# A mixture-of-experts pair of layers on one core: the next layer's gate taken from eight extra columns of the second product

## The chip, the cores and the metric

## The reference

All sizes are fixed: batch 2, sequence 5056, width D = 256, so N = 10112 tokens; E = 8 experts with hidden width F = 1024. All data is fp32.

```python
# 1. gated recurrence over time, per channel
f = lb + (1 - lb) * sigmoid(f_logit);  h = f * h + (1 - f) * x;  y[:, t] = h
# 2. first expert layer: router on normalised rows
logits = (x / |x|) @ (emb / |emb|).T / tau
out = gate * (relu(x @ w1[e]) @ w2[e])          # e = argmax(logits), gate = softmax at e
# 3. second expert layer: router on the first layer's output
logits = x @ w_gate                             # x is the output of layer 1, w_gate is 256 x 8
out = gate * (relu(x @ w1b[e]) @ w2b[e])
```

The output of the first expert layer for one token is a scalar gate times `h @ w2[e]`, where h is the hidden row of 1024. The second router multiplies this by `w_gate`.

## The kernel before, in words

**Stage A, the recurrence.** The tokens go by in 20 chunks of up to 512. TensorE turns the rows of x and f_logit (L1210), VectorE scans (L389), TensorE turns the result back (L1223) and forms the first router's logits with 8-column matmuls (L1229). SyncE loads four chunks ahead and stores the rows.

**The first sort (`routing`, one on each engine).** VectorE finds each token's expert, TensorE counts with ones matrices (L1256, L1259; VectorE waits for them before the scans of L440), and then ten steps of up to 8 tiles each build a table that says which token stands in which slot. In each step VectorE makes one-hot tiles (`one_hots`), ScalarE scales one (`scaled`, L1085), and TensorE multiplies (`chunk`, L1247, 79 matmuls in all). The table gives 47 pairs of 128-slot tiles per layer, each pair of one expert. GpSimd gathers the rows of a pair, and the weights of the first pair are split while the table is finished.

**The pairs (`step`).** 47 pairs belong to the first expert layer and 47 to the second. Each weight and each activation is split into a high and a low part (fp32r), and each product is the sum of three. A pair takes in four quarters j: `up` is 12 matmuls of 256 columns (L1313) and `down` is 12 (L1331), so 48 + 48 for the pair. ScalarE makes the high parts (`split_w1_hi`, `split_w2_hi`, `m_hidden`), VectorE the low parts. `down` of quarters 2 and 3 is issued in the next step. `m_y` (L1141) scales the result into `yb`, and SyncE stores it.

**The second router, before.** Only in the first layer, each of the two tiles of a pair is turned again by two transposes (`turn_y`, L1351), copied by ScalarE (`m_yT`, L1148), multiplied with `w_gate` by two fp32 matmuls of 8 columns (`y_logits`, L1342; each stands as two records in the trace), and the 8 logits are copied by VectorE (`m_logits`, L690).

**The second sort (`resort`).** It runs in small portions, one at each `tick`, beside the pairs: part 0 for the first 32 pairs' tokens, part 1 for the rest. `FRONT` is the number of portions before the table steps.

Every engine's order of work is the order in which the code is written. The order between engines is kept by semaphores. Bank numbers: 0 and 1 take `up`, 4 the turned input, 5 the second router, 6 and 7 `down`.

## Time and profile before

| what | value |
|---|---|
| median of 3 runs | 1382.06 us (1380.33 to 1382.55) |
| the profiled execution: its time | 1380.53 us |
| its span, first to last instruction | 1378.8 us |
| TensorE busy | 1326.5 us, 96% |
| VectorE, ScalarE, GpSimd busy | 971.3, 836.0, 440.5 us |
| mean granted TensorE clock | 0.974 |

Busy time of TensorE holds overlaps and modelled ends, so the starts of rows are the safer measure of its pace. A row of the timeline gives the start, the time from the first start to the last end, the engine, the line, the operation with its tiles, and how many instructions the row merges. "Idle before" stands in brackets with what ended it. The stages are: stage A to 110 us, the first sort to 166 us, the pairs of the first layer, then the pairs of the second, and the last scatter at the end.

### The profile page before, as it was taken

How to read it: one execution, taken by the hardware profiler on the slowest of the kernel's cores; microseconds unless marked ns; L12 is line 12 of the kernel's file. 1: busy time of each engine (PE TensorE's matmuls, PEld its weight loads, DVE VectorE, ACT ScalarE, POOL GpSimd, SP SyncE). 2: the span in 40 equal slices, each digit the busy share in tenths (PEclk: the TensorE clock that was granted, in tenths of full speed). 3: DMA queues.
4: the chain of work that ended last, by engine and by line, in shares of the span. 5: the costliest groups of instructions: out<-in, count | busy, mean ns of one | idle time of the engine just before them, and what ended most of it. 6: DMA issues, size and time to landing. Idle time of an engine off the chain costs nothing.

```text
span 1378.8 us, 31340 instructions
## 1 busy us (share of the span) xinstructions
PE 1326.5 (96%) x11005; PEld 1296.1 (94%) x11005; DVE 971.3 (70%) x1468; ACT 836.0 (61%) x1402; POOL 440.5 (32%) x458
## 2 busy tenths in 40 slices
PE   7994799999999999999999999999999999999996
PEld 6892499999999999999999999899999999999996
DVE  5888476666666666679876679777777777777773
ACT  5774266666666666666656665556666666666663
POOL 4572222121121221222112144324444444444431
PEclk9995599999999999999999999999999999999998
DMA  7984686656665665668856657446666666666650
GB/s 275 327 273 93 90 260 198 202 199 193 217 198 191 210 199 195 199 204 142 262 157 201 212 194 229 162 154 221 221 217 213 222 224 217 224 214 217 223 185 1
DMA packets 189559, 276.83 MB, mean 201 GB/s; under 512 B 33351, under 2 KB 151765, under 8 KB 189493
## 3 DMA queue, kind: packets, MB, share of 16 engines
q1 hardware_dynamic: 175956, 240.74, 56.5%
q0 software_dynamic: 13536, 35.21, 7.7%
q8 instruction: 41, 0.67, 0.2%
q14 instruction: 26, 0.20, 0.0%
HBM read 242.69 MB, written 35.18 MB: 202 GB/s over the span
## 4 chain that ended last, share of the span: by engine, by line
PE 89%; DVE 6%; issue 2%; POOL 1%; ACT 1%; DMA 1%; SPq 0%; DVEq 0%; POOLq 0%; ACTq 0%
PE bank L1313 38%; PE bank L1331 37%; PE bank L1247 4%; PE bank L1297 3%; PE bank L1342 2%; PE bank L1351 1%; PE bank L1229 1%; PE bank L1210 1%; PE bank L1223 1%; DVE hT L389 1%; DVE gx L379 1%; DVE w1l L363 1%; POOL fg L894 1%; DVE hl L675 0%; DMA fin<-in_f_logit 0%
## 5 line engine op out<-in xcount | busy, mean ns | idle before, releaser
L1313 PE MATMUL bank<-xs,w1h 128*128 128x256 f32 x3008 | 570.3, 288 | 1.5 <-DVE xs L664 1.5
L1125 ACT ACTIVATE hh<-bank 128x512 fp32r<-128x512 f32 x376 | 225.3, 599 | 413.2 <-PE bank L1313 385.1
L1313 PEld LDWEIGHTS bank<-xs,w1h 128*128 128x128 f32 x3008 | 461.3, 189 | 3.2 <-DVE xs L664 1.9
L675 DVE SCALAR_TENSOR_TENSOR hl<-bank,hh 128x512 fp32r<-128x512 f32 x376 | 259.9, 691 | 249.3 <-ACT hh L1125 246.3
L1331 PE MATMUL bank<-w2h,hl 128*128 128x256 f32 x1504 | 423.1, 281 | 0.0
L1331 PE MATMUL bank<-w2l,hh 128*128 128x256 f32 x1504 | 422.4, 281 | 0.0
L1331 PE MATMUL bank<-w2h,hh 128*128 128x256 f32 x1504 | 421.7, 280 | 0.0
L1313 PE MATMUL bank<-xs,w1l 128*128 128x256 f32 x1504 | 421.5, 280 | 0.0
L1313 PEld LDWEIGHTS bank<-xs,w1l 128*128 128x128 f32 x1504 | 283.6, 189 | 0.0
L1331 PEld LDWEIGHTS bank<-w2h,hh 128*128 128x128 f32 x1504 | 283.3, 188 | 0.0
L1331 PEld LDWEIGHTS bank<-w2l,hh 128*128 128x128 f32 x1504 | 283.0, 188 | 0.0
L1331 PEld LDWEIGHTS bank<-w2h,hl 128*128 128x128 f32 x1504 | 283.0, 188 | 0.0
L363 DVE TENSOR_TENSOR w1l<-w1raw,w1h 128x1024 fp32r<-128x1024 f32 x188 | 230.2, 1225 | 44.7 <-ACT w1h L1038 44.6
L370 DVE TENSOR_TENSOR w2l<-w2raw,w2h 128x1024 fp32r<-128x1024 f32 x188 | 230.2, 1225 | 43.2 <-ACT w2h L1046 28.1
L972 POOL DMA_INDIRECT xb<-rows_a,row_i x94 | 110.1, 1172 | 459.2 <-DVE meta L668 440.9
L982 POOL DMA_INDIRECT out_y<-yb,tok x94 | 125.8, 1338 | 312.2 <-DVE tok L683 282.0
L1038 ACT ACTIVATE w1h<-w1raw 128x1024 fp32r<-128x1024 f32 x188 | 197.5, 1051 | 7.3 <-DMA w1raw<-in_moe_w 7.3
L1046 ACT ACTIVATE w2h<-w2raw 128x1024 fp32r<-128x1024 f32 x188 | 197.6, 1052 | 0.8 <-DMA w2raw<-in_moe_w 0.8
L972 POOL DMA_INDIRECT xb<-rows_b,row_i x94 | 108.9, 1159 | 67.0 <-DVE meta L668 29.7
L1141 ACT ACTIVATE yb<-bank,meta 128x256 f32<-128x256 f32 x188 | 78.7, 471 | 11.4 <-PE bank L1331 4.5
L664 DVE TENSOR_TENSOR xs<-bank,xs 128x512 fp32r<-128x512 f32 x94 | 64.9, 690 | 11.7 <-ACT xs L1119 9.5
L1247 PE MATMUL bank<-vals,lane_oh 128*128 128x124 bf16 (+2 forms) x237 | 59.3, 414 | 10.8 <-DVE vals L519 10.8
(160 smaller groups left out, 1033.8 us busy)
## 6 DMA issues: line engine op xcount, KB each, us to landing
w1raw<-in_moe_w SPq DMA_DIRECT2D x94, 1024.0 KB
w2raw<-in_moe_w SPq DMA_DIRECT2D x94, 1024.0 KB, 5.5
rows_b<-yb SPq DMA_DIRECT2D x94, 128.0 KB, 2.1
xin<-in_x SPq DMA_DIRECT2D x19, 512.0 KB, 5.5
fin<-in_f_logit SPq DMA_DIRECT2D x19, 512.0 KB, 7.2
rows_a<-h_rows SPq DMA_DIRECT2D x19, 512.0 KB, 5.2
xb<-rows_a,row_i POOLq DMA_INDIRECT x94, 4.3
xb<-rows_b,row_i POOLq DMA_INDIRECT x94, 5.5
```

Source lines behind the costliest of these rows:

```text
L363: v.tensor_tensor(w1l[:, par(i), cols], w1raw[:, par(i), cols], w1h[:, par(i), cols].bitcast(fp32), ALU.subtract).then_inc(w1_lo, 1)
L370: v.tensor_tensor(w2l[:, par(i), cols], w2raw[:, par(i), cols], w2h[:, par(i), cols].bitcast(fp32), ALU.subtract).then_inc(w2_lo, 1)
L675: v.scalar_tensor_tensor(hl[:, j, :], bank[j % UB][:, :], 0.0, hh[:, j, :].bitcast(fp32), ALU.max, ALU.subtract).then_inc(hid_lo, 1)
L972: pool.indirect_dma_start(xb[:, s, :], None, rows_of(i), bass.IndirectOffsetOnAxis(row_i[:, s:s + 1], 0)).then_inc(x_in[s], 16)
L982: pool.indirect_dma_start(out, bass.IndirectOffsetOnAxis(tok[:, s:s + 1], 0), yb[:, s, :], None, bounds_check=N - 1, oob_is_err=False).the ...
L1038: nc.scalar.activation(w1h[:, par(i), cols], w1raw[:, par(i), cols], ACT.Copy).then_inc(w1_hi, 1)
L1046: nc.scalar.activation(w2h[:, par(i), cols], w2raw[:, par(i), cols], ACT.Copy).then_inc(w2_hi, 1)
L1125: nc.scalar.activation(hh[:, j, :], bank[j % UB][:, :], ACT.Relu).then_inc(hid_hi, 1)
L1141: nc.scalar.activation(yb[:, s, :], bank[Y_BANK + par(i)][:, t * D:(t + 1) * D], ACT.Copy, scale=meta[:, bass.ds(in_layer(i).value(2 * G, ...
L1247: ins = mm(bank[b][:, 0:2 * W], lane_oh[:, g % RS, :, t], vals[:, g % RS, 0:2 * W, t], start=first and t == 0, stop=last and t == w - 1)
L1313: ins = mm(bank[j % UB][:, f * GW:(f + 1) * GW], w[:, p, o:o + P], xs[:, p, a, c * GW:(c + 1) * GW], start=k == 0, stop=k == 3 * DC - 1)
L1331: ins = mm(bank[Y_BANK + p][:, t * D:(t + 1) * D], a[:, j, f * GW + t * P:f * GW + (t + 1) * P], w[:, p, o:o + D], start=(j, t, f, k) == ( ...
```

## The change

The product of each expert's `w2` (1024 x 256) with `w_gate` (256 x 8) is formed once, in the first sort. The result, 1024 x 8 per expert, goes to DRAM (`gates_d`) and is loaded for each pair of the first layer beside `w2`, is split into a high and a low part, and stands as columns 256 to 263 of `w2h` and `w2l`. The 48 `down` matmuls of a first-layer pair have 264 columns instead of 256, and the extra 8 columns are the second router's logits before the gate factor. `turn_y`, `m_yT` and `y_logits` are gone, and `m_logits` copies both tiles' logits from `yb` at once.

The work of the first sort is cut into 16 units, two per expert. A unit is `turn_w2`, 8 transposes of 128 columns, two ScalarE copies of 512 columns (`keep_turned`), and `gate_w2`, 8 fp32 matmuls of 8 columns. Four units are begun ahead of the counting matmuls (`EARLY`), six between these and the table (`SPREAD`), one after each third table step, and the rest behind the table. Seven of the eight `w2` matrices are loaded from the last chunks of stage A on, in addition to the weights of the first pair, and the eighth after the store of the pair table. The first pair's weights are split by ScalarE behind the table steps, where before they were split ahead of them.

Since `down` now takes four banks (4 to 7), `resort` counts and builds its table in one bank (2), by 4 experts at a time in part 0 and by 2 in part 1; both parts begin one step earlier, and `FRONT` of part 1 goes from 15 to 19.

```diff
+    DX = D + E
+    EW = FC * E
+    WUNITS = 2 * E
+    EARLY, SPREAD = 4, 6
...
+        w2_stage = [sb(f"w2_stage{n}", [P, WE], fp32, gate_only) for n in range(5)]
+        w2_turn = sb("w2_turn", [P, 2 * DC * 512], fp32, gate_only)
...
-        X_BANK, L_BANK, Y_BANK = 4, 5, 6
-        CUM_BANK, SUM_BANK = 2, 3
+        S_BANK, X_BANK, Y_BANK = 2, 3, 4
+        w2_all = [w1raw[:, 1, :], w2raw[:, 1, :]] + w2_stage + w2_stage[0:1]
+        T_BANK, TAB_BANK = [5, 7], 4
+        W_BANK = [6, S_BANK]
...
-                if i.var is None and i.const * JS + j >= XA * JS + 2 * JS:
-                    next(part0 if i.const < NP + 2 else part1, None)
+                if i.var is None and i.const >= XA + 1:
+                    next(part0 if i.const < NP + 1 else part1, None)
...
-        FRONT = [18, 15]
+        FRONT = [18, 19]
+        EXPERTS_AT_ONCE = [4, 2]
...
+                if i.var is None and NCH - 5 <= i.const < NCH - 1:
+                    load_all(i.const - (NCH - 5))
                 if i.var is None and i.const == NCH - 1:
+                    load_all(4)
                     load_w1(Index(0))
                     load_w2(Index(0))
+                    load_all(5)
+                    load_all(6)
...
+            load_all(E - 1)
+            store_gates(0)
+            sp.wait_ge(gate_out, 16)
+            load_wg(Index(0))
             sp.wait_ge(dve_c, mark["experts"])
             read_expert(Index(1))
+            sp.wait_ge(w2_turned, 4 * DC)
             load_w1(Index(1))
             load_w2(Index(1))
+            load_wg(Index(1))
...
+            def keep_turned(u):
+
+                wait(act, gate_ok, u - 1)
+                for c in range(DC):
+                    act.wait_ge(w2_turned, 2 * u + c + 1)
+                    o = (2 * (u % 2) + c) * 512
+                    nc.scalar.activation(w2_turn[:, o:o + 512], bank[T_BANK[c]][:, :],
+                                         ACT.Copy).then_inc(w2t_ok, 1)

...
+                for u in range(EARLY):
+                    keep_turned(u)
                 act.wait_ge(lg_ok, NCH)
                 act.wait_ge(shift_ok, 2)
                 nc.scalar.activation(ex[:, 0:TT, :], shifted[:, 0:TT, :], ACT.Exp).then_inc(act_s, 1)
+                for u in range(EARLY, EARLY + SPREAD):
+                    keep_turned(u)
+                    if u == EH * 2:
+                        keep_gates(0)
+                u = EARLY + SPREAD
                 for q, t0 in enumerate(range(0, TT, RC)):
                     scaled(q, min(RC, TT - t0), ST)
+                    if q % 3 == 2:
+                        keep_turned(u)
+                        u += 1
+                for c in range(DC):
+                    split_w1_hi(Index(0), c)
+                for u in range(u, WUNITS):
+                    keep_turned(u)
+                for half in range(2):
+                    split_w2_hi(Index(0), half)
+                keep_gates(1)
...
+                    n = DX if layer_of(i) == 0 else D
+                    nc.scalar.activation(yb[:, s, 0:n], bank[Y_BANK + s][:, 0:n], ACT.Copy,
                                          scale=meta[:, bass.ds(in_layer(i).value(2 * G, 2 * t), 1)]
                                          ).then_inc(y_ok, 1)
-
-            def m_yT(i, t):
-
-                wait(act, y_turned, i.value(G, t + 1))
-                nc.scalar.activation(yT[:, t, :], bank[L_BANK][:, 0:D], ACT.Copy).then_inc(yT_ok, 1)
...
+            def turn_w2(u):
+
+                e, h = divmod(u, 2)
+                if u == 0:
+                    pe.wait_ge(rows_ok, NCH)
+                if h == 0:
+                    pe.wait_ge(all_in[e], 16)
+                for c in range(DC):
+                    wait(pe, w2t_ok, 2 * (u - 1) + c + 1)
+                    for n in range(FC // 2):
+                        o = (h * (FC // 2) + n) * D + c * P
+                        ins = nc.tensor.transpose(bank[T_BANK[c]][:, n * P:(n + 1) * P],
+                                                  w2_all[e][:, o:o + P], ident[:, :])
+                    ins.then_inc(w2_turned, 1)
+
+            def gate_w2(u):
+
+                e, h = divmod(u, 2)
+                pe.wait_ge(w2t_ok, 2 * u + 2)
+                if u == 0:
+                    pe.wait_ge(lg_kept, NCH)
+                if u == EH * 2:
+                    pe.wait_ge(dve_c, mark["totals"])
+                for n in range(FC // 2):
+                    for c in range(DC):
+                        o = (2 * (u % 2) + c) * 512 + n * P
+                        col = (e % EH) * EW + (h * (FC // 2) + n) * E
+                        ins = mm(bank[W_BANK[e // EH]][:, col:col + E], w2_turn[:, o:o + P], wg_T[:, c, :],
+                                 start=c == 0, stop=c == DC - 1)
+                ins.then_inc(gate_ok, 1)
+
+            def gate_step(u):
+                if u < WUNITS:
+                    turn_w2(u)
+                if u > 0:
+                    gate_w2(u - 1)
...
             def routing():
                 T = TT
+                for u in range(EARLY):
+                    gate_step(u)
                 pe.wait_ge(dve_c, mark["oh"])
                 for b in range(2):
 
...
                     ins = mm(bank[2 + b][:, 0:EH * T], ones_b[:, :], oh[:, b * EH:(b + 1) * EH, 0:T],
                              start=True, stop=True)
                 ins.then_inc(pe_s, 1)
+                for u in range(EARLY, EARLY + SPREAD):
+                    gate_step(u)
+                u = EARLY + SPREAD
                 for q, t0 in enumerate(range(0, T, RC)):
-                    chunk(q, min(RC, T - t0), ST, 4, q == 0, t0 + RC >= T)
+                    chunk(q, min(RC, T - t0), ST, bank[TAB_BANK][:, 0:2 * ST], q == 0, t0 + RC >= T)
+                    if q % 3 == 2:
+                        gate_step(u)
+                        u += 1
+                for u in range(u, WUNITS + 1):
+                    gate_step(u)
...
+                n = DX if layer_of(i) == 0 else D
                 for t in range(G):
                     for f in range(2):
                         k = 0
                         for a, w in ((hh, w2h), (hh, w2l), (hl, w2h)):
-                            o = (2 * j + f) * D
-                            ins = mm(bank[Y_BANK + p][:, t * D:(t + 1) * D],
-                                     a[:, j, f * GW + t * P:f * GW + (t + 1) * P], w[:, p, o:o + D],
-                                     start=(j, t, f, k) == (0, 0, 0, 0), stop=(j, f, k) == (JS - 1, 1, 2),
-                                     skip_group_check=True)
+                            ins = mm(bank[Y_BANK + rows_slot(i, t)][:, 0:n],
+                                     a[:, j, f * GW + t * P:f * GW + (t + 1) * P], w[p][:, 2 * j + f, 0:n],
+                                     start=(j, f, k) == (0, 0, 0), stop=(j, f, k) == (JS - 1, 1, 2))
                             k += 1
...
-            def y_logits(i, t):
-
-                wait(pe, yT_ok, i.value(G, t + 1))
-                for c in range(DC):
-                    ins = mm(bank[L_BANK][:, D:D + E], yT[:, t, c * P:(c + 1) * P],
-                             wg_T[:, c, :], start=c == 0, stop=c == DC - 1)
-                ins.then_inc(ylg_ok, 1)
-
-            def turn_y(i, t):
-                s = rows_slot(i, t)
-                wait(pe, y_ok, i.value(G, t + 1))
-                wait(pe, ylg_kept, i.value(G, t))
-                for c in range(DC):
-                    ins = nc.tensor.transpose(bank[L_BANK][:, c * P:(c + 1) * P],
-                                              yb[:, s, c * P:(c + 1) * P], ident[:, :])
-                ins.then_inc(y_turned, 1)
```

How TensorE's instructions move. First the place between stage A and the first pair, before. Rows are in the order of issue; the number at the end is how many follow each other.

```order
L1223 MATMUL bank<-ident,hT 128x128 x6
L1229 MATMUL bank<-en_T,hT 128x8 x6
L1256 MATMUL bank<-oh,upto 128x316 x2
L1259 MATMUL bank<-oh,ones_b 128x316 x2
L1247 MATMUL bank<-vals,lane_oh 128x188 x79
L1297 MATMUL bank<-ident,xb 128x128 x4
L1313 MATMUL bank<-xs,w1h 128x256 x2
L1313 MATMUL bank<-xs,w1l 128x256
```

The same place after the change, its beginning: L1340 and L1346 are the former L1223 and L1229, L1412 and L1415 the counting matmuls (L1256, L1259), L1369 is `turn_w2` and L1385 is `gate_w2`.

```order
L1340 MATMUL bank<-ident,hT 128x128 x6
L1346 MATMUL bank<-en_T,hT 128x8 x6
L1369 MATMUL bank<-ident,w1raw 128x128 x16
L1385 MATMUL bank<-wg_T,w_turn 128x8 x8
L1369 MATMUL bank<-ident,w2raw 128x128 x8
L1385 MATMUL bank<-wg_T,w_turn 128x8 x8
L1369 MATMUL bank<-ident,w2raw 128x128 x8
L1385 MATMUL bank<-wg_T,w_turn 128x8 x8
L1412 MATMUL bank<-oh,upto 128x316 x2
L1415 MATMUL bank<-oh,ones_b 128x316 x2
L1369 MATMUL bank<-ident,w_stage 128x128 x8
L1385 MATMUL bank<-wg_T,w_turn 128x8 x8
```

Two units' transposes now stand together at the start, and three units of `gate_w2` stand ahead of the counting matmuls, for which VectorE waits. Then the table steps after the change (L1401 is the former L1247):

```order
L1401 MATMUL bank<-vals,lane_oh 128x188 x24
L1369 MATMUL bank<-ident,w_stage 128x128 x8
L1385 MATMUL bank<-wg_T,w_turn 128x8 x8
L1401 MATMUL bank<-vals,lane_oh 128x188 x24
L1369 MATMUL bank<-ident,w_stage 128x128 x8
L1385 MATMUL bank<-wg_T,w_turn 128x8 x8
L1401 MATMUL bank<-vals,lane_oh 128x188 x24
L1369 MATMUL bank<-ident,w_stage 128x128 x8
L1385 MATMUL bank<-wg_T,w_turn 128x8 x8
L1401 MATMUL bank<-vals,lane_oh 128x188 x7
L1369 MATMUL bank<-ident,w_stage 128x128 x8
L1385 MATMUL bank<-wg_T,w_turn 128x8 x8
```

The 79 table matmuls are cut into 24, 24, 24 and 7. Behind the last 7 stand three `turn_w2` and four `gate_w2` in all, of which the last two rows here are the first, and then the first pair's input is turned.

The second place is a first-layer pair, where a quarter's `down` ends and the next `up` begins. Before:

```order
L1331 MATMUL bank<-w2h,hh 128x256
L1331 MATMUL bank<-w2l,hh 128x256
L1331 MATMUL bank<-w2h,hl 128x256
L1342 MATMUL bank<-wg_T,yT 128x8 x2
L1313 MATMUL bank<-xs,w1h 128x256 x2
L1313 MATMUL bank<-xs,w1l 128x256
```

After, at the corresponding place (L1496 is the former L1331, L1476 the former L1313):

```order
L1496 MATMUL bank<-w2h,hh 128x264
L1496 MATMUL bank<-w2l,hh 128x264
L1496 MATMUL bank<-w2h,hl 128x264
L1476 MATMUL bank<-xs,w1h 128x256 x2
L1476 MATMUL bank<-xs,w1l 128x256
```

The 8-column matmuls between `down` and `up` are gone, as are the transposes of L1351 at the other quarters, and the `down` matmuls are wider.

## Rows read from the trace of the kernel before

**Rows 1.** Page, parts 1 and 4: engines' busy time; the chain that ended last.

```profile
PE 1326.5 (96%) x11005; PEld 1296.1 (94%) x11005; DVE 971.3 (70%) x1468; ACT 836.0 (61%) x1402; POOL 440.5 (32%) x458
PEclk9995599999999999999999999999999999999998
PE 89%; DVE 6%; issue 2%; POOL 1%; ACT 1%; DMA 1%; SPq 0%; DVEq 0%; POOLq 0%; ACTq 0%
```

**Rows 2.** Timeline of TensorE, input transposes in layer 1, then layer 2.

```profile
260.78 0.60 PE L1297 MATMUL bank<-ident,xb 128*128 128x128 f32 x4
273.88 0.60 PE L1297 MATMUL bank<-ident,xb 128*128 128x128 f32 x4
...
1099.81 0.60 PE L1297 MATMUL bank<-ident,xb 128*128 128x128 f32 x4
1111.59 0.60 PE L1297 MATMUL bank<-ident,xb 128*128 128x128 f32 x4
```

**Rows 3.** Groups of TensorE by line: records of the second router.

```profile
L1342 PE MATMUL bank<-wg_T,yT 128*128 128x8 f32 x376 | 47.7, 235 | 0.0
L1351 PE MATMUL bank<-ident,yb 128*128 128x128 f32 x188 | 35.7, 271 | 0.0
```

**Rows 4.** Timeline of TensorE, 172 to 175 us: first and last of 12 `down` matmuls.

```profile
172.72 0.28 PE L1331 MATMUL bank<-w2h,hh 128*128 128x256 f32 x1
...
174.02 0.28 PE L1331 MATMUL bank<-w2h,hl 128*128 128x256 f32 x1
```

**Rows 5.** Timeline of TensorE, the first sort.

```profile
106.09 1.52 PE L1223 MATMUL bank<-ident,hT 128*128 128x128 f32 x6 [1.04 <-ACT sq L1069]
107.40 2.57 PE L1229 MATMUL bank<-en_T,hT 128*128 128x8 f32 x12
116.75 0.70 PE L1256 MATMUL bank<-oh,upto 128*128 128x316 bf16 x2 [6.79 <-DVE oh L427]
...
128.53 26.92 PE L1247 MATMUL bank<-vals,lane_oh 128*128 128x188 bf16 x79 [10.54 <-DVE vals L519]
...
164.10 0.69 PE L1297 MATMUL bank<-ident,xb 128*128 128x128 f32 x2 [0.84 <-DMA xb<-rows_a,row_i]
166.28 0.80 PE L1313 MATMUL bank<-xs,w1h 128*128 128x256 f32 x2 [1.48 <-DVE xs L664]
```

**Rows 6.** Windows: busy time and count by engine, granted clock, DMA.

```profile
104.00:106.00 2.00, 1.05 (x10) 0.96 (x9) 1.87 (x4) 1.94 (x9) 0.30 (x1) 0.79 0.01 4
106.00:108.00 2.00, 1.91 (x10) 1.94 (x10) 0.00 (x0) 0.36 (x1) 0.00 (x0) 0.50 0.56 190
...
148.00:150.00 2.00, 2.00 (x8) 0.87 (x6) 0.00 (x0) 0.00 (x0) 0.00 (x0) 0.50 0.00 0
...
170.00:172.00 2.00, 2.00 (x19) 2.00 (x18) 1.74 (x3) 1.72 (x3) 0.18 (x1) 1.00 1.11 369
```

**Rows 7.** Timeline of TensorE, the start of stage A.

```profile
8.33 1.08 PE L1210 MATMUL bank<-ident,xin 128*128 128x128 f32 x4 [1.02 <-DMA fin<-in_f_logit]
9.21 1.06 PE L1210 MATMUL bank<-ident,fin 128*128 128x128 f32 x4
...
16.73 1.04 PE L1223 MATMUL bank<-ident,hT 128*128 128x128 f32 x8
17.60 1.85 PE L1229 MATMUL bank<-en_T,hT 128*128 128x8 f32 x16
19.30 0.63 PE L1210 MATMUL bank<-ident,xin 128*128 128x128 f32 x4
```

**Rows 8.** Timelines of VectorE and ScalarE in and behind the first sort.

```profile
118.09 0.81 DVE L440 TENSOR_TENSOR_SCAN before<-ones_f,bank 128x316 f32<-128x316 f32 x1
...
164.83 0.60 ACT L1119 ACTIVATE xs<-bank 128x512 fp32r<-128x512 f32 x1 [18.35 <-PE bank L1297]
```

**Rows 9.** Page, part 6: DMA issues, count, size of each, us to landing.

```profile
w2raw<-in_moe_w SPq DMA_DIRECT2D x94, 1024.0 KB, 5.5
```

**Rows 10.** Timeline of TensorE, a table step of the second sort.

```profile
901.31 1.95 PE L1247 MATMUL bank<-vals,lane_oh 128*128 128x124 bf16 x8
902.91 0.59 PE L1313 MATMUL bank<-xs,w1h 128*128 128x256 f32 x2
```

More of the change, by code:

```diff
@@ L228, in build @@
         w2_in = [sem(f"w2_in{n}") for n in range(2)]
+        all_in = [sem(f"all_in{n}") for n in range(E)]
+        w2_turned = sem("w2_turned")
+        w2t_ok = sem("w2t_ok")
+        gate_ok = sem("gate_ok")
+        gate_kept = sem("gate_kept")
+        gate_out = sem("gate_out")
+        wg_in = [sem(f"wg_in{n}") for n in range(2)]
+        wg_hi = sem("wg_hi")
+        wg_lo = sem("wg_lo")
         w1_hi = sem("w1_hi")
@@ L695, in _ @@
             m_x(Index(0))
+            split_wg_lo(Index(0))
             def step(i):
-                last, last2, nxt = i.plus(-1), i.plus(-2), i.plus(1)
-                if here(last2) and layer_of(last2) == 0:
-                    m_logits(last2, 0)
+                last, nxt = i.plus(-1), i.plus(1)
                 if here(i):
@@ L725, in step @@
                         split_w2_lo(nxt, 1)
+                    if here(nxt) and layer_of(nxt) == 0:
+                        split_wg_lo(nxt)
+                if here(last) and layer_of(last) == 0:
+                    m_logits(last)
                 tick(i, 3)
@@ L1088, in routing @@
             def routing():
-                for c in range(DC):
-                    split_w1_hi(Index(0), c)
-                for half in range(2):
-                    split_w2_hi(Index(0), half)
+                for u in range(EARLY):
+                    keep_turned(u)
                 act.wait_ge(lg_ok, NCH)
@@ L1175, in step @@
                         split_w2_hi(nxt, 0)
-                if here(last) and layer_of(last) == 0:
-                    m_yT(last, 0)
                 tick(i, 2)
@@ L1239, in _, with chunk @@
             a_back(Index(NCH - 1), tiles_in(NCH - 1))
-            def chunk(g, w, W, b, first, last):
+            def turn_w2(u):
[30 more added lines that the diff above has]
+                    gate_w2(u - 1)
+            def chunk(g, w, W, table, first, last):
                 pe.wait_ge(lane_ok, g + 1)
@@ L1325, in down @@
                     wait(pe, y_ok, i.value(G, -G))
+                    if layer_of(i) == 0:
+                        wait(pe, wg_lo, i.value(1, 1))
+                n = DX if layer_of(i) == 0 else D
                 for t in range(G):
@@ L1360, in step @@
             def step(i):
[L1361 removed]
+                last, nxt = i.plus(-1), i.plus(1)
                 if here(i):
@@ L1380, in step @@
                     down(i, 0)
-                if here(last) and layer_of(last) == 0:
-                    turn_y(last, 0)
                 tick(i, 2)
@@ L1386, in step @@
                     down(i, 1)
-                if here(last) and layer_of(last) == 0:
-                    y_logits(last, 0)
                 tick(i, 3)
```

181 lines of the change are left out of this document (112 added, 69 removed).

## The prediction

> **What bounds the kernel now.** I read the page's busy times first, then the chain that ended last, then TensorE's timeline stage by stage, with the granted clock of short windows beside it. The reader is to see that TensorE is busy for 96% of the span and carries 89% of the chain that ended last, with VectorE far behind at 6% [rows 1]. So time is mostly what TensorE is given to do, and the other engines count only where TensorE waits. That is so in one place alone, the first sort. Between the end of the last 8-column matmuls of stage A, at about 109.9 us, and the first `up` matmul at 166.28, TensorE runs 79 table matmuls for 26.92 us and a few small ones, and stands idle for 6.79, then 10.54 us, and again ahead of the first pair [rows 5]. It also runs at the lower of its two clocks there: the granted clock is 0.79 over the window from 104 us, so it falls inside it, is 0.50 at 106 and still at 148, with TensorE busy through the whole window, and is back at 1.00 at 170, some 4 us into dense `up` matmuls [rows 6, 5].
>
> **What goes from the first-layer pairs.** In steady state the input transposes of two following pairs are 273.88 - 260.78 = 13.10 us apart in layer 1 and 1111.59 - 1099.81 = 11.78 us in layer 2 [rows 2]. The two layers run the same 96 wide matmuls, and the difference, 1.32 us, is the second router: four transposes (188 records over 47 pairs) and four 8-column matmuls (376 records, two each) [rows 3], with the wait for the array at each change of kind. TensorE is the limit in both, so all of it is on the path: 47 x 1.32 = 62.0 us go. ScalarE loses two copies a pair and gains one of 64 columns, VectorE exchanges two tiny copies for one and a subtraction of 64 columns. Both engines keep pace with TensorE in layer 2 at 11.78 us a pair and have about the same work as there, so I cost their edits at nothing; if that cover were gone, a late `m_y` would hold the next `down`, and would show as idle time in front of L1496. The gate load is 32 KB a pair beside 2 MB of weights, hidden likewise.
>
> **What comes to the pairs.** 47 x 48 = 2256 `down` matmuls get 8 more columns. Twelve matmuls start between 172.72 and 174.02, that is 11 gaps, 118.2 ns each for 256 columns [rows 4]. At 2.4 GHz 8 columns are 3.3 ns, and by proportion to the gap 3.7 ns. From below the bound is nothing: 256 columns at 2.4 GHz are 106.7 ns, so 11.5 ns of each gap belong to something other than columns and could hold 3.3 more. From above, no row has an fp32r matmul over 256 columns; were the last 8 columns to cost a pass of their own, the nearest row is a record of 8 columns at 0.106 us, 17.60 to 19.30 for 16 of them [rows 7], and 2256 of them 240 us. I take 3.3 ns, 7.5 us in all: it is the columns' own time, and it lies by the proportional value, which rests on the gaps of this very instruction.
>
> The Trainium skill, "TensorE: Matmul & The Clock Gate", section "Back-to-back issue gap", gives columns/2.4 + 2.5 ns, an estimate of 109.2 ns for 256 and 112.5 for 264; the trace's 118.2 does not agree in size, and the difference of 3.3 ns would give the same 7.5 us. By the page's statement on the moving operand, up to 512 columns for all types, the second pass would not come.
>
> **What comes to the first sort.** A unit is 8 transposes and 16 records of 8-column matmuls. At the lower clock six transposes take 107.40 - 106.09 = 1.31 us, 0.218 each, and 12 records take 2.57 us with the last one's own end in it, 0.20 to 0.214 each [rows 5]. A unit is then 8 x 0.218 + 16 x 0.20 = 4.94 us, and 16 units are 79.1 us. At the higher clock it is (17.60 - 16.73) for the transposes and (19.30 - 17.60) for the records, 2.57 us, or 41.1 in all [rows 7]. The four counting matmuls take 1.3 us from 116.75 to VectorE's scan at 118.09 and the table 26.9 us, at the lower clock [rows 5, 8]. TensorE works strictly in the written order, and everything stands ahead of the first pair, so the sum is a chain: 109.9 + 79.1 + 1.3 + 26.9 = 217.2 us. Behind it come the first pair's four transposes at 0.218, the ScalarE copy and the VectorE subtraction, as before: from 164.10, the last two transposes, to 166.28 it was 2.2 us, and two more transposes make 2.6. The first `up` starts at 219.8 instead of 166.28, 53.5 us later.
>
> What lies beside this chain. The counting result comes 9 to 10 us later to VectorE, whose scan began at 118.09 [rows 8]; its chain to the first table step needs 128.53 - 118.09 = 10.4 us, so the first table step is ready near 139, while TensorE is in its units until about 158. The long idle times of before are thus filled and VectorE, ScalarE and GpSimd are covered; the gather of the first rows, which cost TensorE 0.84 us of waiting [rows 5], is covered too. The eight loads of `w2` are 8 MB; one load lands 5.5 us after issue in the median [rows 9], and those for unit 2e have 10 us between them. On SyncE's queue the eighth load waits for the twelfth turned half, and the first gate load for the store of the gates; behind them stand the loads of pair 1, which wait for `experts`. VectorE writes that after the low part of the first pair's `w2`, which now waits for ScalarE behind `keep_turned(15)`: I get 216 us for the issue, 3.5 us ahead of the first `up`, where the trace of before has 3 us. So nothing is late there by more than a fraction of a microsecond. I add 1 us for the 50 or so new waits of TensorE.
>
> **The sum.** -62.0 + 7.5 + 53.5 + 1.0 = 0.0 us. The profiled execution's time of 1380.53 us, of which the span is 1378.8, stays 1380.5. The median of the runs shown, 1382.06, is 1.5 us above it. The sum would give 1382.1 there; I name 1381.0, between the two, because of the clock's short returns (below), of which one of 3 us is as likely as not. What such a kernel's measurement can tell from no change is 0.2%, 2.8 us. So the gain in the pairs is given back in a sort that ran at half clock, and the outcome hangs on three small numbers.
>
> **Rival 1: the clock comes back in the sort.** For it: in stage A the transposes of 8.33 and 9.21 are 0.22 us apart, the lower clock, and those of 16.73 0.11 us, with nothing but transposes (and two tiny ones) run in between [rows 7], so transposes alone brought the clock up; and the first two units' 16 transposes now stand in a row. In stage A a mixture of transposes and 8-column records also kept it. Against it: the table matmuls did not bring it back in 27 us without a gap [rows 5, 6]; a unit has 8 transposes to 16 records, a full chunk of stage A by its code 24 to 16, and the last chunks, where the clock fell, no more input transposes. At full clock throughout, the units are 38.0 us shorter, the counting 0.6, and the table hardly: a 124-column table matmul at full clock takes 1.60/8 = 0.20 us [rows 10], by columns 0.30 for 188 against 0.341, so 3 us. That is 1382.1 - 41.6 = 1340.5 us. Each microsecond spent at the higher clock is one gained, so it decides from 3 us on. I give 0.15 to more than 5 us.
>
> The Trainium skill, same page, "Part 4: PE-mode transpose", says that transposes do not engage the higher clock, which speaks against this rival and for the lower clock throughout. Rows 7 show the opposite for fp32 transposes in this kernel. By the page the first `up` stands at 219.8 us for certain, by the row up to 41.6 us of it can come back.
>
> **Rival 2: the 8 columns are free**, held by the 11.5 ns of each gap. Then it is 7.5 us less, 1374.6 us, still faster by more than 2.8. For it speaks only that gap; against it, that at the lower clock a table matmul of 188 columns takes 0.341 us and at the higher one of 124 columns 0.20 [rows 5, 10], so width is paid for in both. 0.12.
>
> **Rival 3, slower: TensorE waits for ScalarE's copies.** `gate_w2` of a unit needs both copies, and the next but one `turn_w2` the bank. A copy of 512 columns takes 0.60 us [rows 8]. Between the transposes of a unit and its matmuls stand the next unit's transposes, 1.7 us, which cover it; but ScalarE also has the ten scalings of the table and one copy of the gates in the same order, and the records' upper value of 0.214 works in the same direction. A wait of one copy a unit is 16 x 0.60 = 9.6 us, 1391.7 us. It decides from 0.19 us a unit on, a unit of over 5.1 us. 0.16. The second pass of the 8 columns, +240 us, gets 0.02.
>
> **How the numbers follow.** The forecast case has 0.55; its own range is 1376 to 1386, of it 0.13 faster, 0.34 within 0.2%, 0.08 slower. With rival 1 (0.15) and 2 (0.12) faster by over 0.2% is 0.40, within is 0.34, and with rival 3 and the second pass slower is 0.26. The range 1367 to 1391 leaves out most of rival 1 and a little above, under 0.2. It takes in both ends of the records' time (+3.6 us) and of the 8 columns (-7.5 to +0.9 us).
>
> **What would show it.** The first `up` matmul (L1476) at 217 to 221 us, with L1369 at 0.22 and L1385 at 0.20 us a record and the granted clock at 0.50 from about 105 to 223; the first counting matmul (L1412) near 126 to 127; no idle time of TensorE over 1 us between 110 and 217; pairs of layer 1 at 11.78 + 48 x 0.0033 = 11.94 us, those of layer 2 unchanged; gaps of L1496 at 121.5 ns. It is wrong if the windows between 110 and 217 read 1.00 for more than a few microseconds, if the pairs of layer 1 stand at 11.78 or above 12.1 us, or if TensorE shows idle time ahead of L1385, L1401 or L1496.

## The result and the profile after

| | before | after |
|---|---|---|
| median | 1381.74 us (10 runs, 1380.21 to 1382.56) | 1385.62 us (10 runs, 1383.23 to 1387.63) |
| profiled execution, its span | 1380.53, 1378.8 us | 1385.2, 1383.5 us |
| ratio after to before | | 1.0028, 95% interval 1.0018 to 1.0038 |
| mean granted clock | 0.974 | 0.954 |

The change made the kernel slower by 3.9 us. The time lies in the predicted range, but I had named 1381 us, no change, as the likeliest, and the move is beyond the measurement's uncertainty.

The page after, parts 1 and 4. TensorE is busy 30 us longer and carries still more of the last chain [rows 1].

```profile
PE 1356.2 (98%) x10829; PEld 1326.6 (96%) x10829; DVE 974.8 (70%) x1470; ACT 825.5 (60%) x1389; POOL 428.0 (31%) x458
...
PE 91%; DVE 3%; DMA 2%; issue 1%; ACT 1%; POOL 1%; SPq 0%; ACTq 0%; DVEq 0%; POOLq 0%
```

TensorE's timeline of the first sort after, which answers to [rows 5]; columns are start, time, engine, line, operation, count.

```profile
109.56 3.75 PE L1369 MATMUL bank<-ident,w1raw 128*128 128x128 f32 x16
113.11 3.42 PE L1385 MATMUL bank<-wg_T,w_turn 128*128 128x8 f32 x16
116.39 1.95 PE L1369 MATMUL bank<-ident,w2raw 128*128 128x128 f32 x8
...
126.41 0.69 PE L1412 MATMUL bank<-oh,upto 128*128 128x316 bf16 x2
...
152.45 1.95 PE L1369 MATMUL bank<-ident,w_stage 128*128 128x128 f32 x8
154.19 3.42 PE L1385 MATMUL bank<-wg_T,w_turn 128*128 128x8 f32 x16
157.47 8.25 PE L1401 MATMUL bank<-vals,lane_oh 128*128 128x188 bf16 x24
...
217.34 1.09 PE L1460 MATMUL bank<-ident,xb 128*128 128x128 f32 x4
219.91 0.80 PE L1476 MATMUL bank<-xs,w1h 128*128 128x256 f32 x2 [1.48 <-DVE xs L713]
```

There is no idle time left ahead of the table. A unit takes 5.02 us (116.39 to 121.40 in the same timeline), and the first `up` starts at 219.91 us, 53.6 later than before. The windows after show the lower clock in the sort, which answers to [rows 6].

```profile
116.00:120.00 4.00, 4.00 (x21) 4.00 (x21) 1.75 (x3) 1.19 (x2) 2.35 (x2) 0.50 1.05 389
200.00:204.00 4.00, 4.00 (x21) 4.00 (x21) 2.10 (x2) 1.19 (x2) 3.51 (x4) 0.50 0.00 0
```

The input transposes of following pairs after, first two in layer 1 and then two in layer 2 [rows 2].

```profile
404.40 0.60 PE L1460 MATMUL bank<-ident,xb 128*128 128x128 f32 x4
416.35 0.60 PE L1460 MATMUL bank<-ident,xb 128*128 128x128 f32 x4
...
1103.78 0.60 PE L1460 MATMUL bank<-ident,xb 128*128 128x128 f32 x4
1115.60 0.60 PE L1460 MATMUL bank<-ident,xb 128*128 128x128 f32 x4
```

A pair of layer 1 takes 11.95 to 11.98 us (mean 11.967) in place of 13.09, and a pair of layer 2 takes 11.82 in place of 11.785. The first and the last of the 12 wide `down` matmuls of one quarter, which answer to [rows 4]:

```profile
433.07 0.28 PE L1496 MATMUL bank<-w2h,hh 128*128 128x264 f32 x1
...
434.41 0.28 PE L1496 MATMUL bank<-w2h,hl 128*128 128x264 f32 x1
```

That is 1.34 us for 11 gaps. The mean of 87 such quarters between 300 and 560 us is 1.337 us, 121.6 ns a gap, against 1.300 us and 118.2 ns before. To place the rest I read the same transposes at pairs 34, 43, 48, 58 and 93. Before:

```profile
601.20 0.60 PE L1297 MATMUL bank<-ident,xb 128*128 128x128 f32 x4
...
726.92 0.60 PE L1297 MATMUL bank<-ident,xb 128*128 128x128 f32 x4
...
792.38 0.60 PE L1297 MATMUL bank<-ident,xb 128*128 128x128 f32 x4
...
934.84 0.60 PE L1297 MATMUL bank<-ident,xb 128*128 128x128 f32 x4
...
1347.32 0.60 PE L1297 MATMUL bank<-ident,xb 128*128 128x128 f32 x4
```

After:

```profile
619.80 0.60 PE L1460 MATMUL bank<-ident,xb 128*128 128x128 f32 x4
...
737.88 0.60 PE L1460 MATMUL bank<-ident,xb 128*128 128x128 f32 x4
...
797.73 0.60 PE L1460 MATMUL bank<-ident,xb 128*128 128x128 f32 x4
...
938.33 0.60 PE L1460 MATMUL bank<-ident,xb 128*128 128x128 f32 x4
...
1351.97 0.60 PE L1460 MATMUL bank<-ident,xb 128*128 128x128 f32 x4
```

| stretch | before | after | difference |
|---|---|---|---|
| to the first `up` | 166.28 | 219.91 | +53.6 |
| to pair 34 | 434.9 | 399.9 | -35.0 |
| pairs 34 to 43 (part 0 of the second sort) | 125.7 | 118.1 | -7.6 |
| 43 to 48 | 65.5 | 59.9 | -5.6 |
| 48 to 58 | 142.5 | 140.6 | -1.9 |
| 58 to 93 | 412.5 | 413.6 | +1.2 |
| sum | | | +4.7 |

### The profile page after: what moved, and what is told of

The parts are those of the page before. It is cut to its first block, busy times and chain, and to the rows that moved or that the text cites. A ratio compares the mean times of both kernels' runs of the same rounds, so it can differ in the third digit from the quotient of the medians.

```text
span 1383.5 us, 31017 instructions
## 1 busy us (share of the span) xinstructions
PE 1356.2 (98%) x10829; PEld 1326.6 (96%) x10829; DVE 974.8 (70%) x1470; ACT 825.5 (60%) x1389; POOL 428.0 (31%) x458
## 4 chain that ended last, share of the span: by engine, by line
PE 91%; DVE 3%; DMA 2%; issue 1%; ACT 1%; POOL 1%; SPq 0%; ACTq 0%; DVEq 0%; POOLq 0%
PE bank L1476 38%; PE bank L1496 38%; PE bank L1401 4%; PE bank L1385 4%; PE bank L1460 3%; PE bank L1369 2%; DMA w1raw<-in_moe_w 1%; PE bank L1346 1%; PE bank L1327 1%; PE bank L1340 1%; DVE hT L434 1%; DVE gx L424 1%; POOL fg L979 1%; ACT sq L1179 0%; DMA fin<-in_f_logit 0%
## 5 line engine op out<-in xcount | busy, mean ns | idle before, releaser
L1476 PE MATMUL bank<-xs,w1h 128*128 128x256 f32 x3008 | 564.0, 286 | 1.5 <-DVE xs L713 1.5
L1476 PEld LDWEIGHTS bank<-xs,w1h 128*128 128x128 f32 x3008 | 464.8, 189 | 3.0 <-DVE xs L713 1.9
L1496 PE MATMUL bank<-w2h,hh 128*128 128x264 f32 (+1 forms) x1504 | 426.0, 283 | 0.0
L1496 PE MATMUL bank<-w2l,hh 128*128 128x264 f32 (+1 forms) x1504 | 424.8, 282 | 0.0
L1496 PE MATMUL bank<-w2h,hl 128*128 128x264 f32 (+1 forms) x1504 | 424.6, 282 | 0.0
L1476 PE MATMUL bank<-xs,w1l 128*128 128x256 f32 x1504 | 424.3, 282 | 0.0
L1476 PEld LDWEIGHTS bank<-xs,w1l 128*128 128x128 f32 x1504 | 284.5, 189 | 0.0
L1496 PEld LDWEIGHTS bank<-w2l,hh 128*128 128x128 f32 x1504 | 283.7, 189 | 0.0
L1496 PEld LDWEIGHTS bank<-w2h,hh 128*128 128x128 f32 x1504 | 283.0, 188 | 0.0
L1496 PEld LDWEIGHTS bank<-w2h,hl 128*128 128x128 f32 x1504 | 282.6, 188 | 0.0
L1057 POOL DMA_INDIRECT xb<-rows_a,row_i x94 | 99.5, 1058 | 435.5 <-DVE meta L717 417.4
L1262 ACT ACTIVATE yb<-bank,meta 128x264 f32<-128x264 f32 (+1 forms) x188 | 79.3, 474 | 12.7 <-issue 5.8
L1401 PE MATMUL bank<-vals,lane_oh 128*128 128x124 bf16 (+2 forms) x237 | 60.0, 415 | 0.7 <-DVE vals L562 0.7
```

What stands on the lines that cost most here:

```text
L1057: pool.indirect_dma_start(xb[:, s, :], None, rows_of(i), bass.IndirectOffsetOnAxis(row_i[:, s:s + 1], 0)).then_inc(x_in[s], 16)
L1262: nc.scalar.activation(yb[:, s, 0:n], bank[Y_BANK + s][:, 0:n], ACT.Copy, scale=meta[:, bass.ds(in_layer(i).value(2 * G, 2 * t), 1)]).then ...
L1401: ins = mm(table, lane_oh[:, g % RS, :, t], vals[:, g % RS, 0:2 * W, t], start=first and t == 0, stop=last and t == w - 1)
L1476: ins = mm(bank[j % UB][:, f * GW:(f + 1) * GW], w[p][:, o:o + P], xs[:, p, a, c * GW:(c + 1) * GW], start=k == 0, stop=k == 3 * DC - 1)
L1496: ins = mm(bank[Y_BANK + rows_slot(i, t)][:, 0:n], a[:, j, f * GW + t * P:f * GW + (t + 1) * P], w[p][:, 2 * j + f, 0:n], start=(j, f, k) ...
```

## The experiments

Twelve kernels ran. Times are medians, beside runs of the kernel before on the same chip.

**1. The units left out.** `turn_w2`, `keep_turned`, `gate_w2` and the loads for them are removed.

```diff
-                for u in range(EARLY):
-                    gate_step(u)
...
-                for u in range(EARLY, EARLY + SPREAD):
-                    gate_step(u)
...
-                for u in range(u, WUNITS + 1):
-                    gate_step(u)
```

> The changed kernel with all 16 units of the gate product left out of the first sort (turn_w2, keep_turned, gate_w2, and the eight w2 loads for them); the 8 extra columns are filled from 64 columns of w2 per expert, so the router's numbers are not the reference's. Theory A, the units are a chain of TensorE work of 16 x 5.02 us of which idle time of before takes some 24 us: the first input transpose comes at 162 to 164 us as before instead of 217.3, and the whole is 54 us shorter than the changed kernel, 1331.5 us. Theory B, the sort's shift is partly something else (the loads, the later split of the first weights): the first transpose comes after 168 us and the whole is over 1336 us.

Measured: 1334.9 us, ratio to before 0.9655 (0.9639 to 0.9671). The timeline of TensorE has the first input transposes at 165.20 us and the first `up` at 168.88, 2.6 us later than before and 51 to 52 us earlier than in the change:

```profile
165.20 0.66 PE L1430 MATMUL bank<-ident,xb 128*128 128x128 f32 x2 [7.19 <-DVE expert L572]
...
168.88 0.80 PE L1446 MATMUL bank<-xs,w1h 128*128 128x256 f32 x2 [1.48 <-DVE xs L713]
```

Stage A ended 2.5 us later in this execution (a short fall of the clock within it), so the sort itself is as long as before. Without the units the change would be worth 3.4%; the units cost 50.7 us by medians. Theory A holds for the sort. The total is 3.4 us over its forecast by medians and 5.0 in the profiled execution, where 2.5 us are stage A and 2.5 us the stretch from pair 34 to 43 (120.5 us, against 118.1 in the change); number 12 comes back to that stretch.

**2 and 3. More columns in `gate_w2`.** The moving operand, 8 columns of `w_gate`, is repeated 4 or 8 times. The surplus columns are overwritten or unused, the results are the same.

```diff
-                        ins = mm(bank[W_BANK[e // EH]][:, col:col + E], w2_turn[:, o:o + P], wg_T[:, c, :],
+                        ins = mm(bank[W_BANK[e // EH]][:, col:col + 8 * E].rearrange("p (r e) -> p r e", e=E),
+                                 w2_turn[:, o:o + P], wg_T[:, c, :].unsqueeze(1).to_broadcast([P, 8, E]),
                                  start=c == 0, stop=c == DC - 1)
```

> The changed kernel with the moving operand of gate_w2 repeated 4 times, 32 columns instead of 8; the results used are the same. 
Measured with 64 columns: 1366.0 us (1365.57 to 1366.91), ratio 0.9889 (0.9872 to 0.9905). TensorE's timeline of the sort:

```profile
113.93 3.52 PE L1385 MATMUL bank<-wg_T,w_turn 128*128 128x64 f32 x16
117.24 1.91 PE L1369 MATMUL bank<-ident,w2raw 128*128 128x128 f32 x8
118.94 2.23 PE L1385 MATMUL bank<-wg_T,w_turn 128*128 128x64 f32 x16
121.02 1.04 PE L1369 MATMUL bank<-ident,w2raw 128*128 128x128 f32 x8
121.89 1.90 PE L1385 MATMUL bank<-wg_T,w_turn 128*128 128x64 f32 x16
...
194.70 1.11 PE L1461 MATMUL bank<-ident,xb 128*128 128x128 f32 x4 [0.79 <-DVE empty L545]
```

The windows of the same run, clock in the third column from the end:

```profile
120.00:124.00 4.00, 4.00 (x38) 3.92 (x38) 0.00 (x0) 1.70 (x3) 0.01 (x1) 1.00 1.07 359
...
150.00:154.00 4.00, 4.00 (x19) 3.46 (x19) 0.00 (x0) 2.97 (x4) 0.00 (x0) 0.50 1.13 8
```

Eight times the columns cost nothing: 16 records take 113.93 to 117.24, 3.31 us, at the lower clock, against 3.27 with 8 columns, and 1.73 us in the higher one. The clock came up within the second unit, stayed through the following ones, a unit then taking 2.6 us, and fell at the table steps. So the time of a record does not depend on its columns between 8 and 64, and the number of columns decides whether the clock is held; that it is the weights that pace the record is not shown. The gain of 19.6 us over the change is half of theory A's upper bound because the clock is lost at the table steps and comes and goes in the last units. With 32 columns the median of eleven runs is 1375.27 us, and they fall in two groups, seven from 1366.7 to 1377.0 and four from 1387.2 to 1390.3; the ratio of the seven is 0.9939 (0.9922 to 0.9956). The profiled one is of the upper group, and its clock reads 0.50 in the sort:

```profile
120.00:124.00 4.00, 4.00 (x20) 4.00 (x21) 0.00 (x0) 0.56 (x1) 0.66 (x1) 0.50 1.07 363
```

No trace of the lower group was taken. The mean granted clock of each run is on record: 0.962 to 0.969 in the seven and 0.950 to 0.953 in the four, so the seven had the higher clock for longer, most likely in the sort.

**4. One wide product of three.**

```diff
+                            n = DX if layer_of(i) == 0 and k == 0 else D
                             ins = mm(bank[Y_BANK + rows_slot(i, t)][:, 0:n],
```

> The changed kernel with only one of the three down products (high part by high part) 264 columns wide in layer 1, the other two 256: the logits lack the low parts. Theory A, each of 2256 matmuls pays 3.7 ns for its 8 columns: 1504 of them become narrow and the kernel gains 5.6 us, 1380 us, pairs of layer 1 at 11.85 us instead of 11.97. Theory B, the price is not in the columns but in the tiles' layout or the extra bank changes: pairs of layer 1 stay at 11.95 or above, gain under 1.5 us.

Measured: 1383.35 us, ratio 1.0009 (0.9999 to 1.0020). The median is only 2.3 us under the change's, with runs spread from 1379.1 to 1385.1; in the profiled one the stretch from pair 34 to 43 takes 121.9 us, 3.8 more than in the change, which hides most of the gain. The timeline is sharper:

```profile
401.74 0.60 PE L1460 MATMUL bank<-ident,xb 128*128 128x128 f32 x4
...
425.45 0.60 PE L1460 MATMUL bank<-ident,xb 128*128 128x128 f32 x4
```

Two pairs take 23.71 us, 11.86 each, and the mean over some 25 pairs is 11.84. Against 11.967 that is 0.13 us for 32 narrower matmuls, 4.0 ns each. Theory A holds: the columns are paid for, and rival 2 is refuted. The 4.0 ns are not the price of every wide matmul, though. Over the pairs of layer 2 in the same trace, 11.82 us, the 16 that stayed wide cost about 0.02 us, hardly over 1 ns each. All 48 together cost 0.15 us a pair in the change (11.967 against 11.82), 3.1 ns each, and the gaps say 3.4.

**5 and 6. Thirteen units ahead of the table**, with 64 columns and with 8. The units between the table steps go ahead of them.

```diff
-    EARLY, SPREAD = 4, 6
+    EARLY, SPREAD = 4, 9
...
-                    if q % 3 == 2:
-                        gate_step(u)
-                        u += 1
```

> The kernel with 64 columns in gate_w2, with SPREAD = 9 and no units between table steps: 13 units ahead of the table, 3 behind it. Theory A, the granted clock is held by units of 64 columns and lost to table steps: the clock stays at 1.00 from about 120 us to the table, the three moved units take 2.6 us instead of 5.0 each, 7 us less, the first input transpose at 188 instead of 194.7, 1359 us. Theory B, the clock in the units is a matter of chance and of the window in which they fall: the gain of the 64 columns does not grow, 1366 us or more, and the runs spread by over 5 us.

> The changed kernel (8 columns in gate_w2) with the order of the fast variant: 13 units ahead of the table, 3 behind. Theory A, order alone does not bring the clock up, what streams in gate_w2 does: the sum of TensorE's work in the sort stays, first input transpose at 216 to 219 us, 1385 us. Theory B, it is the table steps between units that keep the clock down: the first transpose comes 5 us earlier or more, under 1380 us.

Measured with 64 columns: 1358.75 us, ratio 0.9832 (0.9814 to 0.9849), first transpose at 188.74 us. With 8 columns: 1386.59 us, ratio 1.0028 (1.0016 to 1.0040), no better than the change. Windows of the first (64 columns):

```profile
140.00:144.00 4.00, 4.00 (x40) 4.00 (x38) 1.15 (x3) 1.91 (x4) 0.00 (x0) 1.00 0.81 9
160.00:164.00 4.00, 4.00 (x13) 1.71 (x12) 2.06 (x4) 1.26 (x2) 0.00 (x0) 0.50 0.07 18
```

Windows of the second (8 columns), in the same place:

```profile
150.00:154.00 4.00, 4.00 (x21) 4.00 (x20) 0.00 (x0) 1.19 (x3) 0.00 (x0) 0.50 1.89 5
```

So the order alone gains nothing, and with the clock up it is worth 7 us, as theory A said in both. Number 6 has its first transposes at 218.95 us.

**7. Layer 2's 0.035 us a pair: the weights' layout.** The kernel before with separate tiles and rows of 264 elements.

```diff
-        w2h = sb("w2h", [P, 2, WE], f32r)
...
+            w2h.insert(0, sb(f"w2h{n}", [P, FC, DX], f32r))
```

> The kernel before with only the storage of the split weights as in the change: separate tiles per parity, rows of w2h and w2l 264 elements apart, hh and hl between them; all matmuls 256 columns, everything else as before. Theory A, the 0.035 us by which the pairs of layer 2 became longer (11.785 to 11.82) comes from the layout: the period here is 11.82. Theory B, it comes from the two banks of down per pair: the period here stays at 11.785.

Measured in one run: 11.783 us a pair in layer 2, 13.08 in layer 1. It is not the layout.

**8. The banks of `down`.**

```diff
...
+                                ins = mm(bank[Y_BANK + 2 * p][:, t * D:(t + 1) * D],
...
```

> The changed kernel with both tiles of a layer-2 pair in one bank again, as before the change; layer 1 unchanged. Theory A (layout): layer 2 stays at 11.82 us a pair. Theory B (banks): layer 2 is back at 11.785, layer 1 still 11.97, 1.6 us less in all.

Measured in one run: 11.818 us in layer 2, as in the change. It is not the banks; both expected causes of these two experiments are excluded.

The trace of number 8 shows something else. Its first sort is that of the change, with 8 columns in `gate_w2`, and yet the clock came up in it for some 3.6 us:

```profile
130.47 1.85 PE L1387 MATMUL bank<-wg_T,w_turn 128*128 128x8 f32 x16
132.17 1.07 PE L1371 MATMUL bank<-ident,w_stage 128*128 128x128 f32 x8
```

```profile
130.00:134.00 4.00, 4.00 (x37) 4.00 (x35) 3.59 (x14) 2.25 (x4) 0.00 (x0) 0.93 0.14 46
```

It fell again within the next unit of the same kind. In the four other traces with 8 columns, those of the change and of numbers 4, 6 and 11, it reads 0.50 through the whole sort.

**9 and 10. The address of `xs` and the bank of the turned input.** Number 9 changes both in the kernel of number 7, number 10 the banks alone.

```diff
+        apart = sb("apart", [P, 288], fp32)
...
-        X_BANK, L_BANK, Y_BANK = 4, 5, 6
-        CUM_BANK, SUM_BANK = 2, 3
+        X_BANK, L_BANK, Y_BANK = 3, 5, 6
+        CUM_BANK, SUM_BANK = 2, 4
```

> The kernel before with the weights' layout of the change, the activations xs moved to the address that they have in the change (1152 bytes further), and the turned input in bank 3 as in the change. Theory A, the addresses or the bank of the turned input make TensorE's pairs 0.035 us longer: layer 2 at 11.82 us a pair, layer 1 at 13.11. Theory B, neither: layer 2 stays at 11.785.

> The kernel before with the weights' layout of the change and the turned input in bank 3 instead of 4, with xs at its old address. Theory A, the address of xs and what lies behind it makes the pairs longer: layer 2 is at 11.785 us here. Theory B, the bank does: 11.81.

Number 9, the timeline's transposes in layer 2:

```profile
1101.81 0.60 PE L1304 MATMUL bank<-ident,xb 128*128 128x128 f32 x4
1113.62 0.60 PE L1304 MATMUL bank<-ident,xb 128*128 128x128 f32 x4
```

Number 10:

```profile
1098.80 0.60 PE L1303 MATMUL bank<-ident,xb 128*128 128x128 f32 x4
1110.58 0.60 PE L1303 MATMUL bank<-ident,xb 128*128 128x128 f32 x4
```

By means over 31 pairs, 11.813 and 11.783 us. The whole of number 9 is 3.7 us longer than that of number 10 (1383.18 and 1379.44, one run each). What lies behind the padding, from the constants to `xs` and `yb`, moved by 1152 bytes (and `yT` went elsewhere), and that makes a pair 0.03 us longer. Which tile it is was not tested, but the traces say in which matmuls the time lies: the 12 `up` matmuls of a quarter, which read `xs`, take 1.441 us in number 9 and 1.433 in number 10, the 12 `down` matmuls 1.424 in both (from first start to the start of what follows, means of over 120 quarters in layer 2). From the kernel before to the change `up` went from 1.438 to 1.444 in the same way, and `down` in layer 2 stayed at 1.42.

**11. Part 0 of the second sort one step later.**

```diff
-                if i.var is None and i.const >= XA + 1:
+                if i.var is None and i.const >= XA + 2:
```

> The changed kernel with part 0 of the second sort begun one step later, as before the change. Theory A, the 2.5 us that this part cost more than before come from TensorE's waits for VectorE (0.8 us for the one-hot tile, 0.7 for the first vals), which follow from the shorter step, not from the earlier begin: the steps 34 to 42 again cost 10.4 us over the plain pair, no change in all. Theory B, the earlier begin collides with something in that step: the excess is back at 7.9 us, 2.5 us less.

Measured in one run: 1387.97 us; pairs 34 to 43 take 118.36 us, as in the change (118.08). The begin is not the cause. That the waits follow from the shorter step is not tested by this.

**12. TensorE's part of the second sort one quarter later**, in the kernel of number 5.

```diff
                 lo, hi, T, W, p0, pairs = part_of(r)
-                for _ in range(5):
+                for _ in range(6):
                     yield
                 for b, e, k, number in groups(r):
```

> The kernel with 64 columns and 13 units ahead of the table, and TensorE's counting and table steps of both parts of the second sort one quarter later. Theory A, the excess of part 0 is partly TensorE's two waits for VectorE (0.8 us for the one-hot tile, 0.7 for the first vals): both vanish and steps 34 to 42 take about 116.9 us instead of 118.5, the whole 1.5 us less, 1357.2 us. Theory B, the waits only move to another instruction (VectorE then waits for the counts or the table and is late later): 118 us or more, no gain.

Measured: 1355.69 us (1352.16 to 1360.82), ratio 0.9801 (0.9775 to 0.9826). Pairs 34 to 43 take 116.09 us, and TensorE shows no wait in that part of the trace. This is the fastest of the kernels that compute the reference's result, 26.8 us under the kernel before; its gain over number 5, 3 us by medians, is within the overlap of the two intervals. The stretch is 2.4 us shorter than in number 5, in one trace each. In the nine traces of the change and of numbers 1 to 6, 8 and 11, all without number 12's edit, it takes 118.1 to 121.9 us, so 116.1 is below all of them.

What makes these nine differ stands in pair 38 and just ahead of it. SyncE stores the second sort's `pair` tile (`rows_b<-pair`), and the load of `w1` issued behind it, here in the change and then before, takes long to issue:

```profile
649.27 7.47 SPq L815 DMA_DIRECT2D w1raw<-in_moe_w  x1
...
644.02 7.76 SPq L765 DMA_DIRECT2D w1raw<-in_moe_w  x1
```

ScalarE then waits for these weights, first in the change and then in number 3:

```profile
666.55 1.06 ACT L1123 ACTIVATE w1h<-w1raw 128x1024 fp32r<-128x1024 f32 x1 [0.81 <-DMA w1raw<-in_moe_w]
...
646.93 1.06 ACT L1123 ACTIVATE w1h<-w1raw 128x1024 fp32r<-128x1024 f32 x1 [4.00 <-DMA w1raw<-in_moe_w]
```

VectorE waits for ScalarE (1.0 us in the change, 4.2 in number 3), then works without a gap until it has made the first `vals`, and TensorE waits for these (0.7 and 2.0 us). All nine traces have the wait for `w1`, 0.8 to 4.0 us. The kernel before has none: its ScalarE uses these weights 19.4 us after the start of their issue, while the change asks for them 16.5 us after it and gets them after 17.3. Number 12 has no wait for weights either, so it takes away both waits of TensorE without telling their causes apart.

## Why the prediction was wrong

**The sort: right, the last tenth by luck.** I had the first `up` at 219.8 us and found 219.91. The clock was at 0.50 throughout, the first counting matmul at 126.41. The units took 1.1 us more than forecast (5.02 against 4.94 each), and an earlier end of stage A, the counting and the table took 0.9 less. The 1 us for new waits was not needed.

**Rival 1, the clock's return: did not occur in the profiled execution.** Its time of 1340 us was out of reach in every run with 8 columns. Numbers 3 and 5 show what decides: TensorE is busy without a gap through the units ahead of the table in each of these sorts, and with 64 columns in place of 8 the clock comes up and stays until the table. With 8 columns a short return is possible, as number 8 shows, one in five traces; I had called one of 3 us "as likely as not" and taken 1.1 us off the sum for it. That put the named time 1.1 us too low and is a small part of the miss.

**The pairs: the step that failed.** I cost the edits of VectorE and ScalarE at nothing, because "both engines keep pace with TensorE in layer 2", and took layer 2 as unchanged. The pairs should have given -54.5 us and gave -49.0. Two pieces make up 5.3 of the 5.5 us.

First, part 0 of the second sort. Over nine pairs the plain difference of 1.126 us would give 10.1; it gave 7.6, so 2.5 us went. The wait list of TensorE, 560 to 960 us, after (total, times, longest):

```profile
PE bank L1439 <- DVE oh L599: 0.8, 1, 0.8
PE bank L1401 <- DVE vals L562: 0.7, 1, 0.7
```

Before, two such waits were 0.3 us each. Pair 35, with the first wait, is 1.1 us longer over a plain pair than its like before, pair 38, with the second, 0.9, and the table steps 0.5 in all. For the first wait the timelines show why. Before, the one-hot tile, a 2.6 us operation of VectorE, was ready at 628.42 us and the counting began at 628.48; the router's four records of 8 columns stood between the input transposes (627.39) and the counting and filled most of the time. After, the transposes stand at 631.75, the tile is ready at 632.99 and the counting begins at 633.13: VectorE is the last to end here, and what TensorE no longer does has become idle time. Behind the second wait stand the weights of the pair, which come 0.8 us late, as told at number 12. That the shorter pairs are the reason of both is read from the traces and was not tested by itself. Number 12 takes both waits away and has the stretch 2.0 us shorter than the change and 2.4 shorter than number 5; number 11 shows that the begin has no part in it. My cover was read from pairs without the second sort.

Second, every pair is some 0.03 us longer than forecast, 2.8 us over 94: 11.967 against 11.94 in layer 1, 11.82 against 11.785 in layer 2. It lies in the `up` matmuls, and numbers 7 to 10 tie it to where tiles lie in memory. I had taken the period of layer 2 before as the floor of both layers.

The missing 5.5 us, less the 1.0 us that I added for new waits and with 0.1 of the sort, are but for rounding the 4.7 us by which the profiled executions differ, where the sum had 0.0.

**The 8 columns: right.** I took 3.3 ns, 7.5 us; the gap grew from 118.2 to 121.6 ns, 3.4 ns and 7.6 us in all, and I had forecast 121.5. The 4.0 ns of number 4 hold for the matmuls narrowed there.

**Rival 3**, a wait for ScalarE's copies, did not occur: no idle time of TensorE stands ahead of L1385. The kernel is slower by another way than the one that I priced. One of my signs of being wrong did come, idle time ahead of L1401, but in the second sort, where I had not looked for it.

**The transposes and the clock.** By the Trainium skill, "TensorE: Matmul & The Clock Gate", Part 4: PE-mode transpose, transposes do not engage the higher clock. In number 3 the clock is up with transposes for a third of the time and padded matmuls for the rest, which does not decide it. [rows 7] stay the evidence against, by the spacing of the transposes alone (0.22, then 0.11 us): the profile's granted clock reads 1.00 in those windows from 6 us on, so it does not show the lower level there.

## What to carry to other kernels

Up to 64 columns an fp32 matmul took the same time here as with 8, and filling them brought the clock up and halved the time of the transposes and small matmuls around; the table matmuls stayed as they were. So work moved into a stretch at the lower clock is to be priced at that clock, and then it is worth a try to make it dense: here that turned a loss of 0.3% into a gain of 1.7 to 2.0%. When a step of a pipeline gets shorter, look for the longest operation of each other engine, and for the slowest load, that used to fit into it, and look in the steps that carry extra work and not only in the plain ones.

## What was not expected of the hardware

- A fp32 matmul record of 8, 32 or 64 moving columns takes the same time, about 0.205 us at the lower clock (64 columns: 0.207) and 0.106 to 0.108 at the higher (8 and 64 columns).
- The table matmuls of 188 columns, 0.341 us each at the lower clock before, took 26.9 us for 79 in number 5 as well, though it began at the higher clock, and the clock fell during them. The first 24 of them in number 3 took 8.09 us with some 3 us at the higher clock, against 8.07 at the lower in the change.
- Moving tiles by 1152 bytes in memory changed a pair of dense matmuls by 0.03 of 11.8 us, and the difference lies in the `up` matmuls; over 31 pairs in each trace.
- In numbers 1, 2, 4, 6 and 8 the granted clock fell to 0.50 for about 3.4 us in pair 38, shortly after TensorE had waited 1.3 to 2.0 us. In number 3 the same wait of 2.0 us had no such fall behind it.
